# Router lanes moved from GpSimd to VectorE as two-operand instructions, two row gathers issued a step later, and the last tile's second layer computed in two column halves

## What is computed

```python
scores = scale * q @ k.T, causal; a = softmax(scores); local = a @ v
mem_out = (phi(q) @ M_prev) / (phi(q) @ z_prev)            # phi(x) = elu(x) + 1
x = g * mem_out + (1 - g) * local                          # 2304 tokens x 512
e_idx = argmax(x @ w_gate); gate_w = softmax(x @ w_gate)[e_idx]
eom = sigmoid(x @ w_output_gate)
out[mask] = gate_w * eom[:, e] * (relu(x[mask] @ w1[e]) @ w2[e])   # mask: e_idx == e
```

## Time and profile before

| | |
|---|---|
| median of 3 runs | 462.83 us (462.77 to 463.34) |
| profiled execution, its own time | 464.11 us |
| its span, first to last instruction | 462.2 us |
| granted TensorE clock, mean | 0.998 of full speed |
| PE busy | 453.9 us, 98% of the span |
| DVE / ACT / POOL busy | 303.8 / 276.9 / 195.3 us |

### The profile page before, as it was taken

The page is one execution under the profiler, slowest core; times in us unless marked ns, Lnnn a source line. Parts: engine busy times, 40 slices in busy tenths (PEclk is TensorE's granted clock), DMA queues, the critical chain, the costliest instruction groups (busy, mean ns, idle before and its releaser), DMA issues.

```text
span 462.2 us, 11671 instructions
## 1 busy us (share of the span) xinstructions
PE 453.9 (98%) x4252; PEld 355.9 (77%) x4252; DVE 303.8 (66%) x780; ACT 276.9 (60%) x622; POOL 195.3 (42%) x192
## 2 busy tenths in 40 slices
PE   8999999999999999999999999999999999999995
PEld 6677777677777777787888888888888888888884
DVE  4889898989999997877222399222237957952220
ACT  5889988999999875344222577222237837832221
POOL 7567776769889846251222111221111312221111
PEclk9999999999999999999999999999999999999999
DMA  7234433567544723647322279410117966600000
GB/s 232 83 113 143 134 105 106 191 200 221 194 119 143 239 58 98 210 124 272 129 69 69 72 242 342 171 38 13 46 48 236 326 238 193 223 1 23 23 24 37
DMA packets 44883, 64.09 MB, mean 139 GB/s; under 512 B 7198, under 2 KB 26142, under 8 KB 44832
## 3 DMA queue, kind: packets, MB, share of 16 engines
q1 hardware_dynamic: 40672, 53.81, 35.2%
q0 software_dynamic: 4160, 9.60, 6.5%
HBM read 56.77 MB, written 10.90 MB: 146 GB/s over the span
## 4 chain that ended last, share of the span: by engine, by line
PE 97%; ACT 1%; issue 1%; DVE 0%; another core or an unknown queue 0%; POOL 0%; ACTq 0%; POOLq 0%; DVEq 0%
PE S L1469 23%; PE S L1652 19%; PE S L1653 18%; PE S L1654 18%; PE STK L1469 4%; PE TP_ps L1469 4%; PE TP_ps L1465 3%; PE TP_ps L1692 2%; PE STK L1465 2%; PE STK L1687 2%; PE S L1465 1%; ACT w_hi0b L778 0%; PE TP_ps L1675 0%; DVE probs L970 0%
## 5 line engine op out<-in xcount | busy, mean ns | idle before, releaser
L749 ACT ACTIVATE probs<-probs,neg_max 128x128 f32<-128x128 f32 (+2 forms) x144 | 82.8, 582 | 5.1 <-DVE neg_max L970 4.5
L695 POOL DMA_INDIRECT out<-x_ring,slot_tok_i x23 | 26.9, 1171 | 134.9 <-ACT x_ring L835 102.9
L1652 PE MATMUL S<-w_hi,x_hi 128*128 128x512 f32 x180 | 70.2, 390 | 0.0
L1654 PE MATMUL S<-w_hi,x_lo 128*128 128x512 f32 x180 | 70.1, 389 | 0.0
L1653 PE MATMUL S<-w_lo,x_hi 128*128 128x512 f32 x180 | 70.0, 389 | 0.0
L618 POOL DMA_INDIRECT x_ring<-x_tokens,slot_tok_i x29 | 32.0, 1105 | 85.2 <-DMA out<-x_ring,slot_tok_i 67.9
L1469 PE MATMUL S<-k_pair,q_pair 64*128 64x256 f32 (+5 forms) x384 | 64.3, 442 | 0.0
L1652 PE MATMUL S<-w_hi0b,hid_hi 128*128 128x512 f32 x152 | 61.7, 406 | 0.0
L970 DVE CUSTOM_DVE_ANT_0 probs<-S,mask 128x128 f32<-128x128 f32 (+3 forms) x128 | 55.1, 487 | 6.8 <-PE S L1469 6.3
L1653 PE MATMUL S<-w_lo0b,hid_hi 128*128 128x512 f32 x152 | 59.4, 391 | 0.0
L1654 PE MATMUL S<-w_hi0b,hid_lo 128*128 128x512 f32 x152 | 59.2, 389 | 0.0
(11 more groups left out here) (230 smaller groups left out, 875.9 us busy)
## 6 DMA issues: line engine op xcount, KB each, us to landing
w_raw<-in_moe_w SPq DMA_DIRECT2D x60, 512.0 KB, 5.3
q_pair<-in_qt SPq DMA_DIRECT2D x15, 288.0 KB, 2.9
k_pair<-in_kt SPq DMA_DIRECT2D x15, 288.0 KB, 3.4
v_nat<-in_v SPq DMA_DIRECT2D x16, 256.0 KB, 3.5
x_tokens<-x_out SPq DMA_DIRECT2D x16, 256.0 KB, 2.4
x_ring<-in_moe_w SPq DMA_DIRECT2D x2, 512.0 KB, 4.9
m_aug<-in_m_aug SPq DMA_DIRECT2D x1, 648.0 KB, 6.6
m_turned<-in_m_t SPq DMA_DIRECT2D x1, 512.0 KB, 3.6
```

The costliest lines, as they stand in the source:

```text
L695: nc.gpsimd.indirect_dma_start(out=out[:, :], out_offset=bass.IndirectOffsetOnAxis(ap=slot_tok_i[:, t:t + 1], axis=0), in_=x_ring[:, t % X ...
L749: last = nc.scalar.activation(pr, pr, ACT.Exp, bias=neg_max[:, slot, h:h + 1], scale=-1.0, accum_out=sums[g % 2][:, at, 0:1])
L1652: T.matmul(dst, hi, part(i, k)[:, cols], start=first, stop=False)
L1654: return T.matmul(dst, lo, part(i, k)[:, cols], start=False, stop=last)
```

## The change

It has five parts. (1) POOL's ten `r_lanes` instructions are gone; DVE writes the lanes of batches 0 and 1 in `routing_between`, a new place between `read_loc` and the masks of slots 3 to 6, in steps 10 to 14, one or two token blocks at a time (two of batch 1 in `routing_ahead(13)`). (2) `lanes` is one `tensor_tensor` over several blocks with both operands broadcast, in place of a `tensor_scalar` for each block; two `tensor_scalar` of `place` become `scalar_tensor_tensor` with a constant column as second tensor, and the cast in `so_far` a `tensor_tensor` maximum of a tile with itself. (3) `so_far(2, 3)` and the first half of `place(2)` move behind `read_loc` of the next step. (4) The gathers of tiles 1 and 2 are issued in step 16, after x of pair 14 is added. (5) The last tile's second layer runs over columns 0 to 255, then 256 to 511, in 48 matmuls of 256 columns, and ACT moves each half by itself. The second half now goes to `O_ps` and waits for the move of the tile before (`y_done`).

```diff
-    LAST_RESULT = S4[:, 0:512]
+    LAST_RESULT = S4[:, 0:DM // 2]
@@ gpsimd
-                for t in range(b * TPB, (b + 1) * TPB):
-                    nc.gpsimd.tensor_scalar(r_lanes[:, t, :], iota_f[:, :], r_lane[:, t:t + 1], None, ALU.is_equal).then_inc(lanes_done, 1)
...
+                    if x == G - 2:
+                        for t in range(1, EARLY_TILES):
+                            gather(t, gather_first[t], LAST * S)
...
-                elif 0 <= g - 9 - KD < 2:
-                    lanes(g - 9 - KD)
...
-                    for t in range(EARLY_TILES):
-                        gather(t, gather_first[t], LAST * S)
+                    gather(0, gather_first[0], LAST * S)
@@ scalar
+            act.wait_ge(last_half, 1)
+            at = ring(total - 1)
+            nc.scalar.activation(x_ring[:, at, 0:DM // 2], LAST_RESULT, ACT.Copy, scale=x_ring[:, at, DM:DM + 1])
             act.wait_ge(y_mm, total)
-            at = ring(total - 1)
-            nc.scalar.activation(x_ring[:, at, 0:DM], LAST_RESULT, ACT.Copy, scale=x_ring[:, at, DM:DM + 1]).then_inc(y_done, 1)
+            nc.scalar.activation(x_ring[:, at, DM // 2:DM], O_ps[:, DM // 2:DM], ACT.Copy, scale=x_ring[:, at, DM:DM + 1]).then_inc(y_done, 1)
@@ vector
-                return V.tensor_copy(r_so_far[:, n, :], s_far[:, n, :])
+                return V.tensor_tensor(r_so_far[:, n, :], s_far[:, n, :], s_far[:, n, :], ALU.max)
...
-                link(V.tensor_scalar(r_part[:, ts], r_slot[:, ts], 0.5 - P / 2, 1.0 / P, ALU.add, ALU.mult))
-                link(V.tensor_scalar(r_tile_of[:, ts, E], r_part[:, ts], ROUND, -ROUND, ALU.add, ALU.add))
+                link(V.scalar_tensor_tensor(r_part[:, ts], r_slot[:, ts], 0.5 - P / 2, per_tile[:, 0:1].broadcast_to([P, TPB]), ALU.add, ALU.mult))
+
+            def place_lanes(b):
+                ts = tiles_of(b)
+                link(V.scalar_tensor_tensor(r_tile_of[:, ts, E], r_part[:, ts], ROUND, less_round[:, 0:1].broadcast_to([P, TPB]), ALU.add, ALU.add))
...
-                for t in range(b * TPB + first, b * TPB + end):
-                    V.tensor_scalar(r_lanes[:, t, :], iota_f[:, :], r_lane[:, t:t + 1], None, ALU.is_equal).then_inc(lanes_done, 1)
+                at = slice(b * TPB + first, b * TPB + end)
+                n = end - first
+                V.tensor_tensor(r_lanes[:, at, :], iota_f[:, None, :].broadcast_to([P, n, P]),
+                                r_lane[:, at][:, :, None].broadcast_to([P, n, P]), ALU.is_equal).then_inc(lanes_done, n)
...
+            def routing_between(g):
+                if g == 10:
+                    lanes(0, 0, 2)
+                elif g == 11:
+                    lanes(0, 2, 4)
+                elif g == 12:
+                    lanes(0, 4, 5)
+                elif g == 13:
+                    lanes(1, 0, 2)
+                elif g == 14:
+                    so_far(2, 3).then_inc(hot_done, 1)
+                    lanes(1, 4, 5)
+                elif g == 15:
+                    place_tiles(2)
...
                 elif g == 13:
                     largest(2)
+                    lanes(1, 2, 4)
...
                 elif g == 15:
+                    place_lanes(2)
                     early_tiles()
-                    lanes(2, 0, 3)
+                    lanes(2, 0, 2)
...
                 elif g == 13:
                     choose(2)
-                    so_far(2, 3).then_inc(hot_done, 1)
                     open_gate(2)
                 elif g == 14:
                     read_ranks(2)
-                    place(2)
                 elif g == 15:
-                    lanes(2, 3)
+                    lanes(2, 2, 5)
...
                     read_loc(x)
+                if valid(g):
+                    routing_between(g)
@@ tensor
-            second_layer(total, range(KF), 1, E - 1, LAST_RESULT)
+            for dst, half in ((LAST_RESULT, 0), (O_ps[:, DM // 2:DM], 1)):
+                if half == 1:
+                    pe.wait_ge(y_done, total)
+                for c in range(KF):
+                    if half == 0 and c % 4 == 0:
+                        pe.wait_ge(hidT_lo[c // 4], total)
...
+                    start = c % 2 * 512 + half * (DM // 2)
+                    last = products(dst, hid_hi[:, c, :], hid_lo[:, c, :],
+                                    (4 + c // 2, slice(start, start + DM // 2)), 1, c == 0, c == KF - 1)
+                last.then_inc((last_half, y_mm)[half], 1)
```

More of the change, by code:

```diff
@@ L128, in memory_attention_top1_moe @@
     void_most = sb("void_most", [P, 1])
+    per_tile = sb("per_tile", [P, 1])
+    less_round = sb("less_round", [P, 1])
     r_void = sb("r_void", [P, E], bf16)
@@ L277, in memory_attention_top1_moe @@
     scale_stored = [sem(f"scale_stored{n}") for n in range(2)]
-    placed = sem("placed")
     lanes_done = sem("lanes_done")
@@ L310, in memory_attention_top1_moe @@
     y_done = sem("y_done")
+    last_half = sem("last_half")
     stored = sem("stored")
@@ L608, in low_ahead @@
                 nc.gpsimd.tensor_tensor(w_lo0[0][:, k, :], raw_piece(0, k), w_hi0[0][:, k, :].bitcast(f32), ALU.subtract).then_inc(lo_first, 1)
-            def lanes(b):
-                pool.wait_ge(r_consts_dve, 1)
-                pool.wait_ge(placed, b + 1)
-                for t in range(b * TPB, (b + 1) * TPB):
-                    nc.gpsimd.tensor_scalar(r_lanes[:, t, :], iota_f[:, :], r_lane[:, t:t + 1], None, ALU.is_equal).then_inc(lanes_done, 1)
             def gather(t, s, rows=N):
@@ L940, in router_consts @@
                 V.memset(void_most[D:P, :], float((EARLY_TILES - 2) * P))
+                V.memset(per_tile[:, :], 1.0 / P)
+                V.memset(less_round[:, :], -ROUND)
                 V.tensor_scalar(desc[:, :], iota_i[:, 0:E], -1.0, float(E), ALU.mult, ALU.add)
@@ L1125, in place, with place_tiles @@
             def place(b):
+                place_tiles(b)
+                place_lanes(b)
+            def place_tiles(b):
                 ts = tiles_of(b)
@@ L1130, in place @@
                 link(V.tensor_reduce(r_slot[:, ts], r_sel[:, ts, :], AX.X, ALU.add))
-                link(V.tensor_scalar(r_part[:, ts], r_slot[:, ts], 0.5 - P / 2, 1.0 / P, ALU.add, ALU.mult))
-                link(V.tensor_scalar(r_tile_of[:, ts, E], r_part[:, ts], ROUND, -ROUND, ALU.add, ALU.add))
[L1133 to L1137, removed]
+                link(V.scalar_tensor_tensor(r_part[:, ts], r_slot[:, ts], 0.5 - P / 2, per_tile[:, 0:1].broadcast_to([P, TPB]), ALU.add, ALU.mult))
+            def place_lanes(b):
+                ts = tiles_of(b)
+                link(V.scalar_tensor_tensor(r_tile_of[:, ts, E], r_part[:, ts], ROUND, less_round[:, 0:1].broadcast_to([P, TPB]), ALU.add, ALU.add))
+                link(V.scalar_tensor_tensor(r_lane[:, ts], r_tile_of[:, ts, E], -float(P), r_slot[:, ts], ALU.mult, ALU.add))
             def lanes(b, first=0, end=TPB):
-                for t in range(b * TPB + first, b * TPB + end):
-                    V.tensor_scalar(r_lanes[:, t, :], iota_f[:, :], r_lane[:, t:t + 1], None, ALU.is_equal).then_inc(lanes_done, 1)
+                at = slice(b * TPB + first, b * TPB + end)
+                n = end - first
+                V.tensor_tensor(r_lanes[:, at, :], iota_f[:, None, :].broadcast_to([P, n, P]),
+                                r_lane[:, at][:, :, None].broadcast_to([P, n, P]), ALU.is_equal).then_inc(lanes_done, n)
             def early_tiles():
@@ L1705, in first_layer, with second_layer @@
                     last.then_inc(hid_mm, 1)
-            def second_layer(n, cs, i, e, dst=O_ps[:, :]):
+            def second_layer(n, cs, i, e):
                 for c in cs:
-                    if c == 0 and dst is not LAST_RESULT:
+                    if c == 0:
                         pe.wait_ge(y_done, n)
@@ L1715, in second_layer @@
                         split_wait(pe, e, 4 + c // 2)
-                    last = products(dst, hid_hi[:, c, :], hid_lo[:, c, :],
+                    last = products(O_ps[:, :], hid_hi[:, c, :], hid_lo[:, c, :],
                                     (4 + c // 2, slice(c % 2 * 512, (c % 2 + 1) * 512)), i, c == 0, c == KF - 1)
@@ L1774, in _ @@
             pe.wait_ge(relu_act, total)
-            second_layer(total, range(KF), 1, E - 1, LAST_RESULT)
+            for dst, half in ((LAST_RESULT, 0), (O_ps[:, DM // 2:DM], 1)):
[4 more added lines that the diff above has]
+                        pe.wait_ge(hidT_lo[c // 4], total)
+                    if half == 0 and c % 2 == 0:
+                        split_wait(pe, E - 1, 4 + c // 2)
+                    start = c % 2 * 512 + half * (DM // 2)
+                    last = products(dst, hid_hi[:, c, :], hid_lo[:, c, :],
+                                    (4 + c // 2, slice(start, start + DM // 2)), 1, c == 0, c == KF - 1)
+                last.then_inc((last_half, y_mm)[half], 1)
 _INS = ["qt", "kt", "v", "m_aug", "m_t", "w_pair", "beta", "moe_w1", "moe_w2"]
```

## The result

The changed kernel has a median of 469.7 us in 6 runs (467.79 to 471.09), beside 463.35 for the kernel before (6 runs, 462.77 to 466.93). The ratio on record is 1.0121, with a 95% interval of 1.0092 to 1.0149 (the two medians alone give 1.0137): slower. The median lies 0.7 above the predicted range. The profiled execution took 468.35, and that of before 464.11.

A forecast was written before the change was run, and what follows sets the result against it. PE, busy 98% of the span, was taken as the bound, so only delays to its matmuls count. Held lanes +4.87, gathers -0.72 and tail +0.28 gave +4.43, forecast 467.2 us, range 462.8 to 469.0.

The forecast's parts named there:

- Held lanes: Steps 10 to 15: DVE's lanes behind read_loc wait until POOL's phi_T ends, so slot 3's masks come late; +4.87 us.
- PE pays in full: Steps 10 to 15: each us by which slot 3's mask comes later than about +2.6 is lost to PE.
- Step 15: Step 15: r_part held to +3.54, mask of slot 3 at +3.57 instead of +2.97; +0.60 us.
- Gathers: Step 16: with two gathers issued later, PE's idle of 0.72 before the next turn_w goes; -0.72 us, bounds 0 to 0.72.
- Tail: Last tile in halves: more matmuls +0.34, wait for hid_lo +0.15, shorter last ACT move -0.21; +0.28 us in all.
- Rival D: Last tile: as the main forecast, but half-width matmuls go at the weight load's 0.188, 3.2 more; 470.4 us, chance 0.04.
- Sum: Whole kernel: 4.87 - 0.72 + 0.28 = +4.43 on the profiled 464.11; 467.2 us after carrying it to the median.
- The range: Total time: 462.8 to 469.0 us, leaving out the no-hold and slow-tail rivals.
- rival B: Steps 10 to 15: no hold comes about, so the kernel is faster by 1.29; 461.5 us, chance 0.16.
- A: The main forecast: lanes held to phi_T's end; 467.2 us, own range about 466.0 to 468.6, chance 0.68.
- rival C: Steps 10 to 15: hold ends 0.71 after phi_T's start, steps +0.63, no change in total; 463.0 us, chance 0.12.
- two SBUF inputs: Steps 10 to 15: a DVE instruction with two SBUF inputs contends with POOL's SBUF reads; the first to start keeps the ports.

The follow-up runs named there:

- e1: The changed kernel with the router's place (the lanes and other moved DVE work) ahead of read_loc instead of behind it; 466.19 us, ratio to before 1.0057.
- e13: The changed kernel with POOL's phi_T waiting in steps 10 to 14 until that step's lanes are written; 466.8 us, ratio to before 1.0075.
- e15: The kernel before with later gathers, so_far(2, 3) and half of place(2) ahead of read_loc, two-operand place, so_far and lanes of batches 2, 3; 462.4 us, ratio 0.9984.
- e8: The kernel before with later gathers, and so_far(2, 3) and the first half of place(2) in old forms ahead of read_loc; 463.44 us, ratio 0.9988.
- e7: The kernel before with only the third gather (tile 2) moved behind the sums of pair 14; 463.37 us, ratio 0.9984.
- e3: The changed kernel with phi_T written from q_exp alone by a one-input tensor_scalar; result differs, so only rows are read: steps 10 to 15 take 1.46 more than before.
- e2: The changed kernel with lanes as one tensor_scalar per token block in the same places; 469.36 us, ratio to before 1.0136.

## Why the prediction was right, and where it was off

The place, the mechanism and the direction were right, as was every large term; the time itself lay outside of my range. Against the profiled executions, which start alike within 0.13:

- **Held lanes.** Masks forecast at +3.69, +3.69, +3.56, +3.69, +3.72 and +3.57 came at +3.70, +3.70, +3.57, +3.69, +3.63 and +3.54. Forecast +4.87, measured +4.56. About half of the 0.31 is in the masks, which came 4.74 later in sum and not 4.87: before, that of step 10 stood at +2.66 where I used +2.62, and the new one of step 14 came 0.09 earlier than forecast. The other half is in "PE pays in full", the mis-sized step: in steps 10 to 14 `values` follow the late mask after 1.95 and followed the early one after 1.99. e1 shows the cause inside one kernel, and e13 by taking `phi_T` away.
- **Step 15, right by another path.** I priced it by its mask, 0.60, and it came out at 0.61. But the end of that step follows the last lanes of batch 2, by 0.56 to 0.58 in all kernels told of here. The held `r_part` moved them with everything behind it on DVE: they are written at +10.90, beside +10.28 before and +10.03 in e15, where `r_part` stands ahead of `read_loc` and runs unheld. e8 tells the two paths apart, with `values` in place and 0.26 lost. That the mask gives nearly the right number is luck.
- **Gathers.** Forecast -0.72, measured -0.76, and -0.79 alone. e7 puts it on the third gather.
- **Tail.** Forecast +0.28. From the first of its matmuls to the end of ACT's last move it takes 6.82 instead of 6.56, +0.26, and all behind step 16 +0.30. The matmuls start 0.12 apart, there is a wait of 0.20 for the low half of `hid`, and ACT's last move takes 0.47 instead of 0.69. Rival D (0.188 apart) fell, though its time, 470.4, is the nearest to the median of all.
- **Sum.** Forecast +4.43 on the profiled execution, measured 468.35 - 464.11 = 4.24. My bounds for the terms (3.0 to 5.6 together) held it.
- **The range.** It missed the median by 0.7 for a reason that no term had: in half of the runs, to go by their times and clocks, the start of the kernel lasts 3 us longer; in the one that was profiled, 1.7 of it comes ahead of the fall of the clock, with a wait for a load, and 1.3 in the stretch at half clock. The kernel before had such runs as well, though not among the three that its first median was taken from.

Two slips in my sums did not matter: 0.13, 0.35 and half of 0.85 are 0.91 and not the 0.85 of rival B, and the upper end of 469.0 is 0.4 above the 468.6 that I gave as A's own, without a working.

Rival B (no hold) fell with the first row of `r_lanes`, rival C (release after 0.71) too; e3 shows that the release of C comes with a one-input `phi_T`, though C's price for the steps does not. What failed in my reasons was on the side. I had named two SBUF inputs as what makes an instruction wait; e2 shows that the one-input form is held just as well, and the row at 104.64 of the kernel before could have told me. The Trainium skill ("SBUF — State Buffer", section "Who interferes with whom") says that `tensor_scalar` can contend by another way, a mode that takes both ports; e2's 1.81 agrees with a hold. That this mode is the reason no run shows: alone, the `tensor_scalar` of 128 columns takes 0.28, no less than the 0.28 or 0.29 of the two-input form. In e1 and e13 I twice took DVE's freedom for granted: without the hold the lanes still do not fit in steps 10 and 13, and POOL's chain, once late, holds DVE elsewhere.

## What to carry to other kernels

Before moving small work from GpSimd to VectorE, lay both engines' timelines side by side at the exact place: what matters is which of GpSimd's instructions is running when the moved one begins, and not how long the moved one is. The same instruction ran at its own length when it began 0.9 us earlier, or late in a one-input instruction, and cost up to 1.0 us of TensorE's time when it began just behind the start of a two-input one. When a change has five parts and its total is lost in the scatter of the start, compare the lengths of equal steps in the traces, which here repeat within 0.05 us. And look at what ends each step: the same delay of VectorE reached TensorE through the masks in five steps and through the last lanes in the sixth.

## What the hardware showed that I had not expected

- Late in a one-input instruction of POOL, DVE's two forms differ: `r_part` of 5 columns as `tensor_scalar`, 1.22 after the start of `q_exp`, took 0.45, to `q_exp`'s end (e8); as `scalar_tensor_tensor` at the same place 0.17 (e15) and 0.16 (e1). So the two-operand form of `r_part` was worth having at that place, though not under a two-input instruction.
- A gather that POOL issued just behind the end of a group of matmuls kept ACT from starting on their result: ACT began 1.75 after the matmuls' end before, 0.30 in e7, where a gather had ended 0.1 ahead of that end. Why it does so no run here shows.
- The start of the kernel has three courses: without a wait for `k_pair`, with it (1.2 us or more later), and with it and over 3 us at half clock (3 us later in all). The clock fell in two of the 13 profiles, and both had waited for that load. What chooses between the courses stays open.
